# Decay table kept in DRAM with the heads side by side, and another order of TensorE's work up to the first rows of attention

## What is computed

```python
# attention: q, k, v are (2, 8, 768, 64); lam is one decay for each of the 8 heads
rel = pos[:, None] - pos[None, :]
Dmask = np.where(rel >= 0, lam[:, None, None] ** rel[None, :, :], 0.0)
for b in range(nb):                      # blocks of tokens
    intra = np.einsum('bhic,bhjc->bhij', qb, kb) * Dmask[None]
    intra = np.einsum('bhij,bhjd->bhid', intra, vb)
    inter = np.einsum('bhid,bhde->bhie', qb * lam_pow[None], kv_state)
    out[:, :, sl] = intra + inter
    kb_dec = kb * rev_pow[None]
    kv_state = lam_block[None, :, None, None] * kv_state + np.einsum('bhsd,bhse->bhde', kb_dec, vb)
# then x = out by token; x = x + FFT mixing, layer norm, relu(un @ w1) @ w2; then one more such layer norm + w3, w4
```

## Time and profile before

| | us |
|---|---|
| three runs, median | 576.14 |
| three runs, lowest and highest | 573.77 and 576.69 |
| the profiled execution, device time | 576.8 |
| the profiled execution, span from first to last instruction | 574.9 |
| TensorE busy in the span | 567.6 |
| mean granted TensorE clock | 1.000 |

### The profile page before, as it was taken

One profiled execution on the slowest core, in us unless ns is written; L12 is line 12 of the kernel. 1 busy time (PEld: TensorE's weight loads), 2 busy tenths in 40 slices (PEclk: granted clock), 3 DMA queues, 4 the chain that ended last, 5 costly groups with the idle time before them and its releaser, 6 DMA issues.

```text
span 574.9 us, 10752 instructions
## 1 busy us (share of the span) xinstructions
PE 567.6 (99%) x4042; PEld 392.6 (68%) x4042; DVE 350.7 (61%) x608; ACT 245.5 (43%) x480; POOL 167.1 (29%) x157
## 2 busy tenths in 40 slices
PE   9999999999999999999999999999999999999997
PEld 5899987665666666666666666666666666666663
DVE  2446899799776776647869576975265533422223
ACT  1245657646763233324456454543232433232231
POOL 2657982375510011021295212620004300000000
PEclk9999999999999999999999999999999999999999
DMA  7999892000157346630235422132000223200001
GB/s 248 355 355 362 305 336 69 2 19 1 20 91 201 113 135 140 146 110 3 74 91 139 119 75 75 38 73 56 1 2 1 55 49 100 74 2 1 0 1 74
DMA packets 78948, 59.08 MB, mean 103 GB/s; under 512 B 39466, under 2 KB 65202, under 8 KB 78260
## 3 DMA queue, kind: packets, MB, share of 16 engines
q1 hardware_dynamic: 76548, 53.64, 32.6%
q10 hardware_dynamic: 1872, 3.21, 1.5%
q0 software_dynamic: 480, 1.57, 0.9%
HBM read 42.94 MB, written 6.30 MB: 86 GB/s over the span
## 4 chain that ended last, share of the span: by engine, by line
PE 84%; DVE 11%; POOL 2%; issue 2%; ACT 1%; DVEq 0%; ACTq 0%; POOLq 0%
PE bank L708 36%; PE bank L688 33%; PE bank L487 3%; PE bank L457 2%; PE bank L498 2%; DVE arena L1380 2%; PE bank L564 2%; DVE arena L1216 1%; PE bank L508 1%; DVE arena L1218 1%; PE bank L470 1%; PE bank L632 1%; DVE arena L1225 1%; DVE arena L1345 1%; DVE arena L1311 1%
## 5 line engine op out<-in xcount | busy, mean ns | idle before, releaser
L708 PE MATMUL bank<-arena 128*128 128x512 f16 x1152 | 287.2, 379 | 0.3
L688 PE MATMUL bank<-arena 128*128 128x256 f16 x2016 | 259.2, 273 | 0.5 <-DVE arena L1218 0.4
L688 PEld LDWEIGHTS bank<-arena 128*128 128x128 f16 x2016 | 196.4, 98 | 75.4 <-DVE arena L1424 1.5
L708 PEld LDWEIGHTS bank<-arena 128*128 128x128 f16 x1152 | 112.4, 98 | 86.9 <-issue 0.8
L1380 DVE SCALAR_TENSOR_TENSOR arena<-arena 128x512 f16<-128x512 f32 x96 | 72.8, 759 | 58.8 <-ACT arena L970 58.6
L970 ACT ACTIVATE arena<-arena 128x512 f16<-128x512 f32 x96 | 60.4, 629 | 103.7 <-DVE arena L1424 98.0
L1418 DVE SCALAR_TENSOR_TENSOR arena<-bank,arena 128x256 f32<-128x256 f32 x48 | 20.2, 420 | 66.5 <-PE bank L688 66.4
L1612 POOL TENSOR_TENSOR arena<-arena 128x512 f32<-128x512 f32 x12 | 18.6, 1575 | 90.0 <-DVE arena L1345 90.0
L1592 POOL TENSOR_TENSOR arena<-arena 128x256 f32<-128x256 f32 x16 | 16.5, 1031 | 83.3 <-DMA arena<-w 64.5
L1024 ACT ACTIVATE arena<-bank 128x256 f32<-128x256 f32 x48 | 18.3, 381 | 49.2 <-PE bank L688 49.2
L1357 DVE TENSOR_TENSOR arena<-arena 128x512 f16<-128x512 f32 x42 | 33.4, 804 | 9.5 <-ACT arena L947 9.3
(11 more groups left out here) (112 smaller groups left out, 527.0 us busy)
## 6 DMA issues: line engine op xcount, KB each, us to landing
arena<-w SPq DMA_DIRECT2D x48, 256.0 KB, 4.3
arena<-w SPq DMA_DIRECT2D x24, 512.0 KB, 4.5
arena<-attn SPq DMA_DIRECT2D x15, 512.0 KB, 5.9
arena<-attn SPq DMA_DIRECT2D x4, 1024.0 KB, 9.9
out<-arena SPq DMA_DIRECT2D x12, 256.0 KB, 2.1
x_near<-arena ACTq DMA_DIRECT2D x6, 256.0 KB, 6.5
x_far<-arena ACTq DMA_DIRECT2D x6, 256.0 KB, 5.7
arena<-c SPq DMA_DIRECT2D x1, 1153.5 KB, 9.0
```

Of the source, the lines that this page charges most:

```text
L688: last = nc.tensor.matmul(bank_, wst[:, i, wx, w, kt, :], xs[s % 2][:, x, ux, :, kt, :], start=not started and k == 0, stop=k == 5, skip_g ...
L708: last = nc.tensor.matmul(ops[t][:], hT[n % 2][:, half, hx, t * P:(t + 1) * P], wdn[:, i, wx, half * DM:(half + 1) * DM], start=first and ...
```

## The change

Four things change, all in the lead-in.

- The table in DRAM is turned round: 256 rows of 8 heads in place of 8 rows of 256. Its rows 1 to 128 are written from `kcol`, the column that ScalarE has copied out of PSUM. Its rows 129 to 255 are zeros, written by a DMA on ScalarE's queue from the zeroed state.
- The masks come in one DMA into a new tile `hankel` (128 partitions, 128 by 8 float32), in runs of 4 KB. VectorE reads it directly for unit (0,0), with a step of 8 elements (32 bytes) from one column to the next. ScalarE splits it with two copies into the old tile `DT`, which all later units read.
- The write of the table now waits for `kcol` and stands ahead of the keys' and the values' loads on SyncE's queue.
- TensorE: 2 empties ahead of the scores, the scores ahead of `powrow`, 2 and 3 empties further on in place of 7 and 7, and the order from the first `keys_values` on is another one. `kcol` and `powrow` swap their PSUM banks.

```diff
-WARM_BEFORE, WARM_BETWEEN, WARM_AFTER = 8, 7, 7
+WARM_BEFORE, WARM_SCORES, WARM_BETWEEN, WARM_AFTER = 8, 2, 2, 3
...
+        hankel = part(148 * KB, P, H)
...
-        powrow_bank, kcol_bank = bank[4], bank[5]
-
-        pow_dram = nc.dram_tensor("pow_dram", [H, PITCH], F32).ap()
+        kcol_bank, powrow_bank = bank[4], bank[5]
+
+        pow_dram = nc.dram_tensor("pow_dram", [PITCH, H], F32).ap()
...
+        def of_parity(table, par):
+
+            return table.rearrange("p n (a r) -> p r a n", r=2)[:, par, :, :]
...
# SyncE
+            sp.wait_ge(kcol_done, 1)
+            sp.dma_start(pow_dram[1:P + 1, :], kcol).then_inc(pow_out, 16)
             load_k(0, k_first)
-            sp.wait_ge(pow_step, 9)
-            sp.dma_start(pow_dram, powers[0:H, :]).then_inc(pow_out, 16)
             load_v(0, v_first)
+            sp.wait_ge(zero_out, 16)
             sp.wait_ge(pow_out, 16)
-            for par in range(2):
-                sp.dma_start(DT[:, par, :, :],
-                             bass.AP(pow_dram.tensor, 1 + par * PITCH, [[1, P], [2 * PITCH, PAIRS], [1, P]])
-                             ).then_inc(mask_in[par], 16)
+            sp.dma_start(hankel.rearrange("p n h -> p (n h)"),
+                         bass.AP(pow_dram.tensor, H, [[H, P], [1, P * H]])).then_inc(mask_in, 16)
...
# TensorE
+            empty(WARM_SCORES, bank[7])
+            scores_of(0, 0, (qk_first[0], 16), None)
+            scores_of(1, 0, (qk_first[1], 16), None)
             for pair in range(PAIRS):
...
             last.then_inc(powrow_made, 1)
-
-            scores_of(0, 0, (qk_first[0], 16), None)
-            scores_of(1, 0, (qk_first[1], 16), None)
             empty(WARM_BETWEEN, bank[7])
             pe.wait_ge(v_first, 16)
             keys_values(0, 0, 0, True)
+            empty(WARM_AFTER, bank[7])
+            pe.wait_ge(kcol_done, 1)
+            rows(0, 0, 0, True)
             keys_values(0, 1, 0, True)
-            empty(WARM_AFTER, kcol_bank)
+            scores_of(0, 1, (qk_second[0], 16), 2)
             pe.wait_ge(powrow_out, 1)
-            rows(0, 0, 0, True)
             rows(0, 1, 0, True)
-            scores_of(0, 1, (qk_second[0], 16), 2)
...
# ScalarE
+            act.wait_ge(zeroed, 1)
+            act.dma_start(pow_dram[P + 1:PITCH, :], state[0][0:PITCH - P - 1, 0, 0:H]).then_inc(zero_out, 16)
...
+            act.wait_ge(mask_in, 16)
+            for par in range(2):
+                nc.scalar.activation(DT[:, par, :, :], of_parity(hankel, par), ACT.Copy).then_inc(mask_made, 1)
+            act.wait_ge(zero_out, 16)
...
# VectorE, in masks(u)
+                if u == 0:
+                    dve.wait_ge(mask_in, 16)
                 for par in range(2):
-                    if u == 0:
-                        dve.wait_ge(mask_in[par], 16)
+                    if u == 1:
+                        dve.wait_ge(mask_made, par + 1)
+                    mask = of_parity(hankel, par) if u == 0 else DT[:, par, :, :]
                     nc.vector.tensor_tensor(PT[b][:, par, :, :], scores[b][par][:].rearrange("p (a n) -> p a n", a=PAIRS),
-                                            DT[:, par, :, :], ALU.mult).then_inc(mask_done, 1)
+                                            mask, ALU.mult).then_inc(mask_done, 1)
```

More of the change, by code:

```diff
@@ L218, in build @@
         lam_in, pow_step, pow_out = sem("lam_in"), sem("pow_step"), sem("pow_out")
-        mask_in = [sem(f"mask_in{par}") for par in range(2)]
+        zero_out, mask_made = sem("zero_out"), sem("mask_made")
+        mask_in = sem("mask_in")
         powrow_made, powrow_out, kcol_made = sem("powrow_made"), sem("powrow_out"), sem("kcol_made")
```

## The result

| | before | with the change |
|---|---|---|
| median of six runs, us | 574.22 | 585.06 |
| lowest and highest | 573.77 and 576.69 | 579.06 and 585.88 |
| profiled execution: device time, span | 576.8, 574.9 | 585.88, 584.0 |
| mean granted TensorE clock of the profiled one | 1.000 | 0.978 |

The changed kernel takes 1.0155 times the time of before, with a 95% interval of 1.0122 to 1.0189: that is 9 us more (10.8 by the two medians). The forecast was 574.9 with a range up to 577.3. It started from 576.14, the median of three runs; the six runs of before in the table have 574.22. No rival describes what happened. The nearest is rival 2 (0.10): the clock is low in the lead-in and in the loop's first units. But there the clock rises late, and here it had risen and fell again.

The account below looks back on a forecast made before the run. TensorE was taken to bound the kernel, with DMA only 0.15 us behind in the loop. A lead-in 1.85 us shorter, capped by DMA to 1.2, took the median from 576.14 to 574.9; range 573.0 to 577.3.

Parts of the forecast that it names:

- rival 2: Lead-in or loop: the clock rises later; 579 if at the lead-in's end, 600 and more within the loop; chance 0.10.
- TensorE behind `kcol`: Lead-in: at a clock slow until about 13, TensorE begins the rows of (1,0) at 20.45, not 22.3, 1.85 us earlier.
- rival 1: Lead-in: the clock rises earlier, at 10.1, loop begins 2.9 us earlier; 574.5 or 573.2 as DMA allows; chance 0.20.
- So I let the keys flow from 7.3: Lead-in loads: keys, values and masks take 1.44 us each at 363 GB/s from 7.3; masks usable at about 12.0.
- Hidden by 2.7 us: Lead-in: keys used from about 9.1, ready at 10.2 and 11.2, before TensorE asks at 12.9 and 16.05.
- the fast level held through the loop, which has no empties: Argument against a later clock rise: the loop kept the 2.4 GHz level without empties.
- 579 if at the end of the lead-in: Price in us of a later clock rise that comes when the lead-in ends.
- my lower bound of 1.9: Lead-in: the table's write costs no less than a small load, 1.9 us, and no more than 4.4.
- VectorE's two masks with a step of 32 bytes: Lead-in: reading `hankel` takes 0.64 to 1.48 us each, about 1.0 taken; hidden if the masks' data are not late.
- ScalarE's two copies: Lead-in: 0.60 us each, twice that if the step costs; done by 15.0, wanted at 17.65, so hidden.
- The gain of 1.2 us: Whole kernel: of TensorE's 1.85 us, the DMA stream lets through 0.55 to 1.35; 1.2 taken.
- rival 3: Up to C1: DMA bytes bind and the later `pv_done` order gives back the masks' saving; 576.1, no change; chance 0.12.

Follow-up runs that it names:

- e1: The changed kernel with 7 and 7 empties in place of 2 and 3; 576.41 us, ratio 1.003.
- e4: The kernel before with TensorE's new order and few empties (2, 2, 3), old table and loads kept; 575.32 us, ratio 1.0028.
- e5: The kernel before with the table's write issued ahead of the keys' load; 575.16 us, ratio 1.0.
- e10: e8 with 9 empties in the last place in place of 4; 575.24 us, ratio 0.9993.
- e7: The kernel before with 2 and 3 empties in place of 7 and 7, nothing else; 576.07 us, ratio 1.0011.
- e3: The changed kernel with TensorE's old order and 7 and 7 empties, new table and loads kept; 576.53 us, ratio 1.0017.
- e9: The kernel before with the table's write first and the keys' and values' loads held back until `kcol` is copied; 575.6 us, ratio 1.0004.
- e8: The kernel before with table's write first, TensorE's new order, 2, 5 and 4 empties, some weight loads behind the next block's queries; 573.71 us, ratio 0.9986.
- e6: The changed kernel with 20 unused 128x256 float16 products ahead of the loop; 581.76 us, ratio 1.0111.
- e2: The changed kernel with the keys' load issued ahead of the table's write; 582.04 us, ratio 1.0127.

## Why the prediction was wrong, step by step

**TensorE behind `kcol`, "at the speeds of now (slow until about 13)".** This step failed first. In the profiled execution the clock was up at 5.8, in e1, e4, e5 and e10 near 10.4. I took the moment of one execution as a property of the kernel. Rival 1 had this case (0.20), and its sum took the masks as the next limit, with the keys in time.

**"So I let the keys flow from 7.3", and "Hidden by 2.7 us".** This failed too. The place of the hole was right, the rate behind it was not: 152 and 135 GB/s for 2 us, not 363. The keys came at 10.75, not 9.1, and the masks at 13.66, not 12.0. TensorE was ready at 9.7 instead of 12.9, and the first unit's keys were ready at 11.9 instead of 10.2: 3.2 and 1.7 us turn the cover of 2.7 into a stop of 2.2.

**The term that is missing: a clock that falls.** The sum and all rivals let the clock rise once and stay. A fall behind a stop was put at nothing, without a reason, and it is what the kernel pays: in the profiled execution the clock was low from 12.7 to 36.6, and the delay is 9.1 us.

**Rival 2: "the fast level held through the loop, which has no empties".** That was the argument against the outcome that came true, and it proves less than I drew from it. A level that holds in the loop says nothing of whether the loop regains it. It stayed at 1.2 GHz for 24 us, the loop's units among them. My price for it, "579 if at the end of the lead-in", was near the best of the six runs (579.06); the others took 582.6 to 585.9. I had also let it come from a late rise alone. In the profiled execution it came from an early rise, a stop, and a fall: rival 1, and then the outcome of rival 2. The price was off by its own terms as well: 6.3 us more on a start 1.85 earlier gives 576.14 - 1.85 + 6.3, or 580.6, not 579. That it was near one run is luck.

**The cause, as far as it is shown.** The 9 us take both halves. The late data: with keys and masks as before and few empties the time is 575.3 (e4, a fall in 3 of 10 runs) or 576.1 (e7, in 7 of 10). The few empties: putting them back and keeping the data late gives 576.4 (e1) and 576.5 (e3), with no fall of note in 20 runs, though e3 stops for 2.02 us. In the change the mean clock is low in all six runs (0.978 to 0.991). The Trainium skill (TensorE: Matmul & The Clock Gate, Part 1, "HAM oscillation") warns of gaps on TensorE that lower its clock, and means longer ones than this. In the trace a gap of 2.20 us was enough for the fall, and e3's gap of 2.02 us shows that the gap alone doesn't decide.

**What held.** The table's write was issued at 5.68 (5.7 predicted), and the read behind it at 7.22, so it took at most 1.5 us, less than my lower bound of 1.9. VectorE's two masks with a step of 32 bytes: the four take 3.29 us, not 2.55, and with 0.64 each for the two later ones about 1.0 each for the first two, as I took. The Trainium skill (Vector Engine (DVE) Microarchitecture Reference, section 5.2, one source hopping by 4 KiB) gave by my estimate some 0.7 us more for the two. The trace agrees, though with a step of 32 bytes (3.29 - 2.55 = 0.74). ScalarE's two copies took 2.18 us together, within the bound of twice the plain one.

**The gain of 1.2 us.** It isn't borne out. Between executions whose clock rose at the same time (e4 and e5) the new order saves 1.04 us at the loop, against 1.85 predicted, and 0.05 at C1, against 1.2. The 2.26 and 1.26 against the profile of before are for the larger part the earlier rise of the clock. And by the runs e4 is 0.3% slower than before, not faster. On this point rival 3 was nearer than the forecast.

**What stays open.** Why the clock's first rise comes at 4 to 6 us in some executions, near 10.4 in others, and at 13 in the one profile of before. Within one kernel the times can fall in groups (e5: five runs from 572.7 to 573.0, seven from 575.1 to 576.9, all at a mean clock of 1.0). That may in part be the moment of the rise, but only one execution of each kernel has a profile, so it isn't shown; and e9, with its rise near 4 and the earliest C1 of all, took 575.6, so something behind C1 differs too. Whether it is the empties ahead of the stop or behind it that hold the clock isn't settled. The change against e3 speaks for those ahead: its clock fell at 12.7, and at that time e3, after much the same stop, hadn't begun its second seven (13.36). But these are two executions, and in e8 the fall came only 1.6 us after the stop, with TensorE at work. Open, too, is why the DMA stream starts slowly; its engines were busy for 0.85 and 0.60 of the two slow windows.

## What to carry to other kernels

A filler that computes nothing can be what carries the clock over a wait; before taking fillers out, look for the longest wait that the new order can have in its best execution, not in the profiled one, and keep filler around it. Price a fall of the clock by the work up to its return, which can be far longer than the wait ahead of it: here two waits of 3.15 us in sum were followed by 24 us at the low level, and cost 9. A load that is issued later than the stream ahead of it ends should be priced at the rate of a restart, not at that of the stream. And compare two orders of work only between executions whose clock rose at the same time: most of what e4 seemed to gain was that.

## What the runs showed of the hardware that I had not expected

- TensorE fully busy isn't enough to bring its clock back soon. It worked without a gap on short float32 products from 14.88 to 36.6 us at 1.2 GHz. The low stretch had no fixed length: 24 us in the change, 17 in e6, 14 in e2 and e7, 3.4 in e8.
- The granted clock reads 1.00 ahead of the first rise, while the durations are those of 1.2 GHz (in e4 32 score instructions 3.79 us, window at 1.00). After a fall it reads 0.50 and agrees with the durations. Ahead of the first rise, durations are the witness.
- After a pause the DMA stream moved 135 to 172 GB/s for about 2 us, with two tables of different shape, before it was back near 400.
- ScalarE's copies from SBUF with a step of 32 bytes took 1.09 us each for 128x512; its plain copy, which reads PSUM, takes 0.60. No run has a plain copy from SBUF beside it.
